# Windowed attention and two feed-forward layers: a moved spare tile, weighted sums begun one step earlier, the input split first in its step, and later softmax pieces over two chunks

## The reference

```python
w = softmax(weight_gen)                      # over the 7 taps
out[s, head] = sum_k w[s, k, head] * x[s - 6 + k, head]   # 24 columns per head, zeros in front
x = out.reshape(8192, 192)
h = x @ w_in;  x = (h * cos(h)) @ w_out      # 192 -> 2048 -> 192
h = x @ w_in2; x = maximum(0.01 * h, h) @ w_out2   # 192 -> 2048 -> 192
```

## Time and profile before

| | us |
|---|---|
| median of 3 runs | 1229.11 (1229.11 to 1229.75) |
| profiled execution | 1229.15 |
| its span, first to last instruction | 1227.3 |
| TensorE busy | 1190.3 |
| VectorE busy | 912.0 |
| ScalarE busy | 735.1 |
| GpSimd busy | 118.8 |

### The profile page before, as it was taken

One profiled execution on the slowest core, in us unless ns is written; L12 is line 12 of the kernel. 1 busy time (PEld: TensorE's weight loads), 2 busy tenths in 40 slices (PEclk: granted clock), 3 DMA queues, 4 the chain that ended last, 5 costly groups with the idle time before them and its releaser, 6 DMA issues.

```text
span 1227.3 us, 23265 instructions
## 1 busy us (share of the span) xinstructions
PE 1190.3 (97%) x10188; PEld 1063.9 (87%) x10188; DVE 912.0 (74%) x845; ACT 735.1 (60%) x789; POOL 118.8 (10%) x81
## 2 busy tenths in 40 slices
PE   8899889999999999999999999999999999999998
PEld 6678778888998988899898989988898998989976
DVE  7989797686876768777686877768687676877532
ACT  3766555575756657465565756557575665747544
POOL 4865210000000000000000000000000000000000
PEclk9899989999999999999999999999999999999999
DMA  8121000101001010100101010010100101000000
GB/s 225 52 69 53 33 1 2 46 2 46 1 14 33 1 46 2 46 2 1 46 1 46 1 46 2 1 46 1 46 1 14 34 1 46 1 14 1 1 14 27
DMA packets 10661, 32.68 MB, mean 27 GB/s; under 512 B 836, under 2 KB 5314, under 8 KB 10304
## 3 DMA queue, kind: packets, MB, share of 16 engines
q1 hardware_dynamic: 10560, 31.19, 7.9%
HBM read 24.89 MB, written 6.29 MB: 25 GB/s over the span
## 4 chain that ended last, share of the span: by engine, by line
PE 87%; DVE 6%; POOL 3%; ACT 2%; issue 1%; ACTq 0%; POOLq 0%
PE slot L915 38%; PE acc_a L915 27%; PE acc_b L915 17%; DVE prods L277 2%; DVE g_lo L678 2%; PE slot L1086 2%; ACT g_hi L523 1%; POOL prods L277 1%; POOL prods L271 1%; POOL out_hi_lo L464 0%; DVE prods L271 0%; PE slot L835 0%; POOL out_hi_lo L462 0%; PE slot L848 0%; DVE gate L742 0%
## 5 line engine op out<-in xcount | busy, mean ns | idle before, releaser
L915 PE MATMUL acc_a<-g_hi,out_hi_lo 64*128 64x512 f32 x2000 | 709.1, 394 | 15.4 <-DVE prods L277 15.4
L678 DVE TENSOR_TENSOR g_lo<-gate,g_hi 128x1024 fp32r<-128x1024 f32 x256 | 321.1, 1254 | 197.0 <-ACT g_hi L523 197.0
L915 PEld LDWEIGHTS acc_a<-g_hi,out_hi_lo 64*128 64x128 f32 x2000 | 368.7, 185 | 42.9 <-issue 17.4
L915 PE MATMUL acc_b<-g_hi,out_hi_lo 64*128 64x512 f32 x1000 | 397.6, 398 | 7.1 <-DVE g_lo L678 5.4
L915 PE MATMUL acc_a<-g_lo,out_hi_lo 64*128 64x512 f32 x1000 | 392.6, 393 | 0.0
L915 PE MATMUL acc_b<-g_lo,out_hi_lo 64*128 64x512 f32 x1000 | 392.4, 392 | 0.0
L523 ACT ACTIVATE g_hi<-gate 128x1024 fp32r<-128x1024 f32 x256 | 271.4, 1060 | 130.0 <-PE acc_b L915 111.0
L915 PE MATMUL slot<-x_a_hi,in_a_lo 64*128 64x512 f32 x1000 | 306.8, 400 | 4.0 <-DVE gate L756 3.9
L915 PE MATMUL slot<-x_a_hi,in_a_hi 64*128 64x512 f32 x1000 | 302.6, 393 | 0.0
L915 PE MATMUL slot<-x_b,in_b_hi 64*128 64x512 f32 x1000 | 301.0, 390 | 0.0
L915 PE MATMUL slot<-x_a_lo,in_a_hi 64*128 64x512 f32 x1000 | 299.7, 390 | 0.0
(11 more groups left out here) (98 smaller groups left out, 1121.2 us busy)
## 6 DMA issues: line engine op xcount, KB each, us to landing
x_win<-in_x SPq DMA_DIRECT2D x14, 960.0 KB
out<-result SPq DMA_DIRECT2D x16, 384.0 KB, 2.3
raw_out<-in_moe_w_out SPq DMA_DIRECT2D x1, 1536.0 KB, 17.2
raw<-in_moe_w_out SPq DMA_DIRECT2D x4, 384.0 KB, 3.3
raw_in_a<-in_moe_w_in SPq DMA_DIRECT2D x1, 1024.0 KB, 10.8
raw_in_b<-in_moe_w_in SPq DMA_DIRECT2D x2, 512.0 KB, 13.6
raw<-in_moe_w_in SPq DMA_DIRECT2D x2, 512.0 KB, 5.4
raw<-in_moe_w_in SPq DMA_DIRECT2D x4, 256.0 KB, 3.9
```

Of the source, the lines that this page charges most:

```text
L678: nc.vector.tensor_tensor(g_lo[:, q % 2, :], gate[:, q % 2, :], g_hi[:, q % 2, :].bitcast(FP32), ALU.subtract)\
L915: return nc.tensor.matmul(to, w[rows, :], x[rows, :], start=start, stop=stop)
```

## The change

Six things are edited:

1. `spare`, a tile of one element that ScalarE writes with a sine so that the sine's table is loaded, is allocated last, behind `g_lo`, and no longer between `whole` and `gate`.
2. `scratch` gets a tile of its own (512 elements in each partition) and is no view of `result`; the wait of the first `move_result` on the softmax (`soft_rest`) goes.
3. `ATT_AT` gives the eleven attention instructions to steps 7 to 12 as 2, 1, 1, 2, 2, 3, where it gave 3, 0, 2, 2, 2, 2 to steps 8 to 13.
4. `split_high` and `split_low` of the input of step 16 are issued at the head of step 15, ahead of that step's `g_hi` and `g_lo`, where they were at the head of step 16.
5. The softmax pieces of chunks 3 to 8 and 9 to 15: the sums and reciprocals move from steps 16 and 17 of iteration 1 to step 14 of iterations 1 and 2. Maxima and exponentials stay. Chunk 3's attention waits for the first of the two pieces alone, chunk 9's for the second. On GpSimd the product of the second piece now stands behind `up_of_second(1)` and ahead of `up_of_first(3)`.
6. Behind the last exponential ScalarE takes a one-element sine (`load_sine`), so that the sine's table is loaded there.

```diff
--- before.py
+++ after.py
@@ -199,12 +199,11 @@
         result = sb("result", [P, J, dim])
         ident = sb("ident", [P, P])
         whole = sb("whole", [P, 2, PAIR * N], INT32)
-        spare = sb("spare", [1, 1])
         gate = sb("gate", [P, 2, PAIR * N])
         g_hi = sb("g_hi", [P, 2, PAIR * N], FP32R)
         g_lo = sb("g_lo", [P, 2, PAIR * N], FP32R)
-
-        scratch = result[:, :, :].rearrange("p j d -> p (j d)")[:, 0:per_part * heads]
+        scratch = sb("scratch", [P, per_part * heads])
+        spare = sb("spare", [1, 1])
 
         slots = [ctx.enter_context(nc.psum_tensor(f"slot{n}", [P, PAIR, N], FP32))
                  for n in range(SLOTS)]
@@ -253,10 +252,11 @@
         stored = sem("stored")
 
 
-        ATT_AT = [0] * 8 + [3, 0, 2, 2, 2, 2]
+        ATT_AT = [0] * 7 + [2, 1, 1, 2, 2, 3]
 
         ATT_DVE, ATT_POOL = 4, [3, 4]
         ATT_STEPS = 11
+        SOFT_CHUNKS = (C + 3) // 2
         ATT_MULTS = 9
 
         def attention(c, engine):
@@ -279,8 +279,8 @@
 
             def start():
 
-                if c == 3:
-                    engine.wait_ge(soft_rest, 4)
+                if c in (3, SOFT_CHUNKS):
+                    engine.wait_ge(soft_rest, 3 if c == 3 else 4)
                 if c == 0:
                     engine.wait_ge(x_zeroed, batch)
                 engine.wait_ge(x_loaded, [48, 96][c] if c < 2 else 96 + 16 * (c - 1))
@@ -346,9 +346,9 @@
 
 
         SOFT_ROWS = [slice(a * J * heads, b * J * heads)
-                     for a, b in ((0, 1), (1, 3), (3, (C + 3) // 2), ((C + 3) // 2, C))]
-
-        MAX_STEPS, EXP_STEPS, SUM_STEPS = (8, 9), (12, 12), (16, 17)
+                     for a, b in ((0, 1), (1, 3), (3, SOFT_CHUNKS), (SOFT_CHUNKS, C))]
+
+        MAX_AT, EXP_AT, SUM_AT = [(1, 8), (1, 9)], [(1, 12), (1, 12)], [(1, 14), (2, 14)]
 
         def softmax_operands(n):
 
@@ -494,14 +494,21 @@
             for n in (2, 3):
                 pool.wait_ge(soft, 11 + n)
                 pool.tensor_tensor(*softmax_operands(n), ALU.subtract).then_inc(soft_rest, 1)
-            for n in (2, 3):
+            def softmax_last(n):
                 pool.wait_ge(soft, 11 + 3 * n)
                 pool.tensor_tensor(*softmax_operands(n), ALU.mult).then_inc(soft_rest, 1)
 
-
-
+            softmax_last(2)
+
+
+
+            pool.wait_ge(soft_rest, 3)
+            up_of_second(1)
+            pool.wait_ge(x2_up_ready, 2)
+            softmax_last(3)
             pool.wait_ge(soft_rest, 4)
-            for c in range(1, C):
+            up_of_first(3)
+            for c in range(2, C):
                 up_of_second(c)
                 if c + 2 < C:
                     up_of_first(c + 2)
@@ -555,8 +562,6 @@
                 act.wait_ge(filled, fills(i, step))
                 if c >= 1:
                     act.wait_ge(stored, c * 16)
-                else:
-                    act.wait_ge(soft_rest, 4)
                 src = slots[step % SLOTS]
                 nc.scalar.activation(
                     result[:, :, 0:DA].rearrange("p j (h c) -> p h j c", h=2),
@@ -603,8 +608,8 @@
                     split_high(i, FIRST_INPUT_STEP, i + 1)
                 if kind(i, step) == "output":
                     move_result(i, step, i - 2)
-                if step == INPUT_STEP and input_splits(i, step):
-                    split_high(i, step, i + 1)
+                if step == INPUT_STEP - 1 and input_splits(i, INPUT_STEP):
+                    split_high(i, INPUT_STEP, i + 1)
                 in_first = kind(i, step) == "first"
                 if in_first:
                     q = UNITS.index(step)
@@ -626,9 +631,14 @@
                     leave_res_a()
                 first_read(i, step)
                 for n in (2, 3):
-                    if (i, step) == (1, EXP_STEPS[n - 2]):
+                    if (i, step) == EXP_AT[n - 2]:
                         act.wait_ge(soft_rest, n - 1)
                         exponentials(n)
+                        if n == 3:
+                            load_sine()
+
+            def load_sine():
+                nc.scalar.activation(spare[:, :], ident[0:1, 0:1], ACT.Sin)
 
             def exponentials(n):
                 rows = SOFT_ROWS[n]
@@ -651,7 +661,7 @@
             exponentials(1)
 
             act.wait_ge(ident_ready, 2)
-            nc.scalar.activation(spare[:, :], ident[0:1, 0:1], ACT.Sin)
+            load_sine()
             act.wait_ge(out_loaded, 16)
             for f in range(0, TILES, 4):
                 nc.scalar.activation(W1.out[:, f:f + 4, 0:dim], raw_out[:, f:f + 4, :], ACT.Copy)\
@@ -730,8 +740,8 @@
                     split_second_low(i, step)
                 slot = slots[step % SLOTS][:, :, :].rearrange("p a n -> p (a n)")
                 in_first = kind(i, step) == "first"
-                if step == INPUT_STEP and input_splits(i, step):
-                    split_low(step, i + 1)
+                if step == INPUT_STEP - 1 and input_splits(i, INPUT_STEP):
+                    split_low(INPUT_STEP, i + 1)
                 if step == FIRST_INPUT_SPLIT and input_splits(i, step):
                     split_low(FIRST_INPUT_STEP, i + 1)
                 if in_first:
@@ -759,9 +769,9 @@
                 if i < LAST:
                     split_second_low(i, step)
                 for n in (2, 3):
-                    if (i, step) == (1, MAX_STEPS[n - 2]):
+                    if (i, step) == MAX_AT[n - 2]:
                         softmax_max(n)
-                    if (i, step) == (1, SUM_STEPS[n - 2]):
+                    if (i, step) == SUM_AT[n - 2]:
                         softmax_inverse_sum(n, 8 + 3 * n)
 
             def iteration(i, spread, steps=STEPS):
```

## The result

| | before | after |
|---|---|---|
| median, us | 1229.16 (1229.11 to 1229.75) | 1185.75 (1185.18 to 1185.97) |
| span of the profiled execution | 1227.3 | 1183.4 |
| mean granted clock | 0.993 | 0.996 |

The way was right and the size was not.

What follows compares the result with a forecast made beforehand. TensorE, busy 97% of the span, was taken as the bound, so gains come only from its waits or lower clock. 1229.15 - 15.3 (steady waits) - 9.2 (iterations 1 and 2) = 1204.6 us; 1200 to 1214 held about 8 in 10.

Steps and rivals of the forecast that it cites:

- 3. The tiles: Placement of `scratch` and `spare` in SBUF: shifts `gate`, `g_hi`, `g_lo` by 32 bytes at most, taken as 0 us.
- another distance of pairs than 0.233: Sign against the forecast: TensorE's matmul pairs starting at some spacing other than 0.233 us.
- 1. The wait of iterations 2 to 14: TensorE's wait for the attention's last add goes entirely: 13 x 1.18 = 15.3 us gained.
- 2. Iterations 1 and 2: Start-up losses of TensorE from waits, restarts and lower clock fall from 14.6 to 5.4 us: 9.2 gained.
- `g_lo` of unit 10: Start-up, VectorE: one more product ahead of this `g_lo` makes TensorE wait 1.35 us, bounds 0 and 3.
- `x_up`: Iteration 2: GpSimd's second product ahead of `up_of_first(3)` makes TensorE wait 0.6 us, bounds 0 and 2.
- the slot behind the exponentials: Start-up, ScalarE: sine's table load delays `g_hi` and Prelu; TensorE waits 1.35 us for the slot, bounds 0.3 and 3.
- The switch of tables: ScalarE's table load counted at 1.28 us without drain; with a drain at both switches the total would be about 1207.
- A: Rival, start-up: new waits in iterations 1 and 2 as long as the old, total 1213.8 us; chance 0.24.
- B: Rival, steady iterations: the wait for the last adds stays, only the start gains, total 1220 us; chance 0.04.
- C: Rival: the wait becomes an equal one for `x1_ready` or `lo_ready`, start loses the gain, 1229 us; chance 0.03.
- D: Rival, slower: early `split_high` holds ScalarE and queues `g_hi`, `g_lo` and a Prelu in 14 iterations, 1237 us; chance 0.03.

Runs made afterwards that it cites:

- e2: The kernel before the change with only `spare` moved to the end, every order as before; 1208.89 us, ratio 0.9836.
- e1: The changed kernel with only `spare` put back between `whole` and `gate`; 1206.41 us.

## Why the prediction was wrong

**The step that failed is "3. The tiles".** It took the moved tile for nothing, and let "1% of the time of TensorE's pairs ... 12 us to either side" stand as what it would be if the address counted. It measured 19.6 (e2) and 20.7 (e1): 0.105 us of a unit's 4.42, 2.4%. The argument was that pairs that read `g` and pairs that read `x` are 0.23 to 0.24 apart alike in the earlier trace rows, which took the pairs of `x`, whose tiles were not shifted, for a measure of undisturbed ones. They are not: they read inputs and weights that lie at the same remainder in before and after, and still the five of a unit take 0.93 in before and 0.91 in after. Equal distances of two sorts can't bound what slows both. Nor do rows of two decimals tell 0.2325 from 0.2273 on two starts. The range was drawn from the schedule's terms and did not take in even the 12 us that the step had named. The text did say that another distance of pairs than 0.233 would show it wrong, and that is what came. Without the moved tile (e1) the time is 1206.41, inside the range of 1200 to 1214.

**1. The wait of iterations 2 to 14: right.** 1.18 us an iteration were forecast, from the starts and not from the wait's 0.93. The weight loads of the attention's transposes give the period: first to last start in iteration 3 and in iteration 14, before,

```profile
L839 PEld LDWEIGHTS slot<-ident,prods x8: 104/108/109, 299.9 to 300.3; 64*64 64x64 f32 x8
...
L839 PEld LDWEIGHTS slot<-ident,prods x8: 106/108/109, 1101.4 to 1101.8; 64*64 64x64 f32 x8
```

and e1, the same placement and the new order:

```profile
L849 PEld LDWEIGHTS slot<-ident,prods x8: 106/108/109, 291.7 to 292.1; 64*64 64x64 f32 x8
...
L849 PEld LDWEIGHTS slot<-ident,prods x8: 108/108/109, 1080.0 to 1080.4; 64*64 64x64 f32 x8
```

801.5 / 11 = 72.86 and 788.3 / 11 = 71.66: 1.20 less. The adds end 2.5 us ahead of the pair that waited for them (2.8 forecast), the split 1.7 ahead of its use (1.7 forecast), `g_lo` at 292.51, 1.6 ahead of the fifth pair behind 292.93 (1.6 forecast).

**2. Iterations 1 and 2: the gain was put too high by some 2 to 3 us.** 9.2 were forecast. From before to e1 the span is 21.4 shorter (1227.3 and 1205.9); 13 x 1.20 = 15.6 of it are the steady waits, and 5.8 are left. By the medians (22.1, and 23.1 from e2 to after) it is 6.5 to 7.5. Against the estimates, in after: `mid_b` 0.9 (0 forecast), `g_lo` of unit 10 2.1 (1.35), `g_lo` of unit 13 1.0 (1.3), `x_up` 1.6 (0.6), the slot behind the exponentials 0 (1.35). The wait of 2.1 comes from these two rows, VectorE and then GpSimd of after:

```profile
126.78 3.96 DVE L688 TENSOR_TENSOR g_lo<-gate,g_hi 128x1024 fp32r<-128x1024 f32 x1
```

```profile
123.49 6.17 POOL L496 TENSOR_TENSOR taps_w<-taps_w,scratch 128x1344 f32<-128x1344 f32 x2
```

I had the add of pairs collide with GpSimd, as it did in the earlier trace rows; with one product more ahead, it is `g_lo` that stands there, 3.96 in place of 1.2, and TensorE waits for that one. And the clock did not stay up, as I let it:

```profile
132.00:138.00 6.00, 6.00 (x41) 4.97 (x41) 5.93 (x6) 3.84 (x4) 0.00 (x0) 0.72 0.01 3
144.00:149.00 5.00, 5.00 (x58) 4.24 (x56) 4.90 (x6) 4.13 (x6) 0.97 (x1) 1.00 0.00 0
166.30:172.60 6.30, 6.30 (x58) 5.29 (x56) 6.30 (x6) 5.60 (x6) 0.00 (x0) 1.00 0.00 0
```

The two stretches of the earlier trace rows are at full clock now, but behind the wait of 2.1 a new one is at 0.72: (1 - 0.72) x 6 = 1.7 us. Waits 5.6, clock 1.7 and four restarts of 0.25 make 8.3 in place of 5.4, 2.9 more. The single prices were within their bounds, without the clock. With the old placement the waits fall otherwise: e1 has waits of 1.1, 1.8, 1.1, 1.0 and 1.4 us in these iterations, 6.4 in all, the third of them for the slot behind the exponentials (1.35 forecast), and its clock stays up. So how this loss divides between waits and clock depends on the placement; that it is above 5.4 holds in both.

**The switch of tables** was rightly counted at the load alone. ScalarE of after:

```profile
137.06 1.28 ACT L645 ACT_TABLE_LOAD   x1
138.35 2.73 ACT L645 ACTIVATE taps_w<-taps_w 128x1344 f32<-128x1344 f32 x2
141.10 1.28 ACT L641 ACT_TABLE_LOAD   x1
142.40 0.20 ACT L641 ACTIVATE spare<-ident 1x1 f32<-1x1 f32 x1
```

The exponentials end at 141.08 and the second load starts at 141.10; the sine starts 0.02 behind its end. The Trainium skill, ScalarE: Activation LUTs, "What ACT_TABLE_LOAD costs", adds a drain of about 1.38 us to each; no such time is between these rows.

**Rivals.** A (1213.8) is the nearest to what the reordering did by itself: 22.1 to 23.1 us lie between its 15.3 and the forecast's 24.5, nearer to the forecast: the start did gain, by 5.8 to 7.5 us, where A has nothing. B and C are ruled out, since the wait is gone and no other stands in its place. D did not come: `g_lo` behind the split was ready in time.

## What to carry to other kernels

Where TensorE is over 95% busy, read the distance of its matmul pairs in a stretch without waits, and print the start address of each tile that it reads: here the pairs were fast only where weights, inputs and gate values started at the same remainder over 256 bytes, and a tile of one element between two of them cost 20 us of 1206. When a diff adds, drops or moves any tile, bound the effect on the fastest-repeating instruction in per cent of its time and put it in the range; other pairs of the same kernel are no control, since a shifted tile slowed pairs that do not read it. Price a wait by the starts of instructions on both sides of it, and look behind each new wait of some 2 us for a lower clock (after had 0.72 over 6 us behind one of 2.1, e1 none behind one of 1.8).
